# Newly placed tokens per expert: summed over the partitions by VectorE in place of a TensorE matmul

## What is computed

```
order = np.argsort(-flat)
for idx in order:
    tok, e = (int(idx) // E, int(idx) % E)
    if assigned[tok] >= 0 or counts[e] >= cap:
        continue
    assigned[tok] = e
    counts[e] += 1
```

## Time and profile before

| | us |
|---|---|
| median of 3 runs | 1106.54 |
| the profiled execution, its own time | 1105.22 |
| span of its instructions | 1103.1 |
| TensorE busy | 1041.5 |
| VectorE busy | 672.5 |
| one round, from a visit to the same visit of the next (497.10 to 610.20) | 113.1 |
| first route, TensorE mostly idle | about 145 to 190 |

### The profile page before, as it was taken

How to read it: one execution, slowest core, us unless ns; L and a number is a source line. 1 busy time by engine, 2 the same in 40 slices (tenths; PEclk the granted TensorE clock), 3 DMA queues, 4 the chain that set the end, 5 groups by cost and what they waited for, 6 DMA issues and landing times.

```text
span 1103.1 us, 20428 instructions
## 1 busy us (share of the span) xinstructions
PE 1041.5 (94%) x7340; PEld 971.1 (88%) x7340; DVE 672.5 (61%) x1965; ACT 344.3 (31%) x659; POOL 133.8 (12%) x159
## 2 busy tenths in 40 slices
PE   6999932999999999999999999999999999999996
PEld 5888821999999999999999999999999999999995
DVE  4665558877477647765677567755775477634211
ACT  3444422422243224322432234223412341224210
POOL 5554301033010011001100110011001100110001
PEclk9999965999999999999999999999999999999998
DMA  9999443312141113212321123122312230314000
GB/s 200 255 236 246 116 134 105 100 55 60 46 124 59 56 50 106 78 48 58 98 86 48 58 87 96 39 67 77 106 39 67 64 119 17 90 50 124 8 1 29
DMA packets 172988, 96.68 MB, mean 88 GB/s; under 512 B 80224, under 2 KB 158048, under 8 KB 172896
## 3 DMA queue, kind: packets, MB, share of 16 engines
q1 hardware_dynamic: 169056, 82.92, 28.7%
q0 software_dynamic: 3840, 12.59, 3.6%
HBM read 82.90 MB, written 12.58 MB: 87 GB/s over the span
## 4 chain that ended last, share of the span: by engine, by line
PE 82%; DVE 3%; issue 1%; POOL 0%; DMA 0%; DVEq 0%; POOLq 0%
PE bank L1200 21%; PE bank L1202 20%; PE bank L1201 20%; PE bank L1279 6%; PE bank L1280 6%; PE bank L1278 6%; PE bank L1195 1%; PE bank L1160 1%; DVE above L865 1%; PE bank L1187 0%; DVE onehot L1001 0%; DMA xg<-xrows,ids 0%; POOL out_dram L747 0%; PE bank L1166 0%; POOL xg L733 0%
## 5 line engine op out<-in xcount | busy, mean ns | idle before, releaser
L1200 PE MATMUL bank<-h2h,resident 128*128 128x384 f32 x768 | 261.2, 340 | 0.0
L1202 PE MATMUL bank<-h2h,resident 128*128 128x384 f32 x768 | 257.8, 336 | 0.0
L1201 PE MATMUL bank<-h2l,resident 128*128 128x384 f32 x768 | 257.4, 335 | 0.0
L1043 DVE TENSOR_TENSOR pf<-bank,gate 128x384 f32<-128x384 f32 x96 | 53.5, 557 | 159.9 <-PE bank L1202 158.9
L1200 PEld LDWEIGHTS bank<-h2h,resident 128*128 128x128 f32 x768 | 144.3, 188 | 3.0
L1201 PEld LDWEIGHTS bank<-h2l,resident 128*128 128x128 f32 x768 | 144.3, 188 | 2.9
L1202 PEld LDWEIGHTS bank<-h2h,resident 128*128 128x128 f32 x768 | 144.1, 188 | 0.0
L777 ACT ACTIVATE ring<-ring_raw 128x512 fp32r<-128x512 f32 x192 | 117.7, 624 | 65.8 <-DMA ring_raw<-in_moe_w_out_dram 41.0
L797 ACT ACTIVATE ph<-pf 128x384 fp32r<-128x384 f32 x96 | 50.4, 525 | 266.1 <-DVE pf L1043 266.1
L1052 DVE TENSOR_TENSOR ring<-ring_raw,ring 128x512 fp32r<-128x512 f32 x192 | 126.4, 684 | 0.0
L793 ACT ACTIVATE gate<-bank 128x384 f32<-128x384 f32 x96 | 47.1, 490 | 172.5 <-PE bank L1202 172.4
(11 more groups left out here) (175 smaller groups left out, 1689.9 us busy)
## 6 DMA issues: line engine op xcount, KB each, us to landing
ring_raw<-in_moe_w_dram SPq DMA_DIRECT2D x128, 256.0 KB, 2.9
ring_raw<-in_moe_w_out_dram SPq DMA_DIRECT2D x64, 256.0 KB, 2.9
qraw<-in_q_dram SPq DMA_DIRECT2D x24, 256.0 KB, 4.5
kraw<-in_k_dram SPq DMA_DIRECT2D x24, 256.0 KB, 5.1
vraw<-in_v_dram SPq DMA_DIRECT2D x24, 256.0 KB, 5.1
xrows<-xrow SPq DMA_DIRECT2D x24, 256.0 KB, 3.8
resident_raw<-in_moe_w_gate_dram SPq DMA_DIRECT2D x12, 256.0 KB, 4.5
resident_raw<-in_moe_w_val_dram SPq DMA_DIRECT2D x12, 256.0 KB, 4.6
```

What stands on the lines that cost most here:

```text
L1043: nc.vector.tensor_tensor(pf[:, f % 2, :], bank[2 * (f % 2) + 1][:, 0:CAP], gate[:, f % 2, :], ALU.mult).then_inc(p_ready, 1)
L1200: nc.tensor.matmul(ps, wh, xhi, start=start, stop=False)
L1201: nc.tensor.matmul(ps, wh, xlo, start=False, stop=False)
L1202: return nc.tensor.matmul(ps, wl, xhi, start=False, stop=stop)
```

## The change

The count step goes. Its DVE part and that of the rank step become one part, `V_RANK` = 8, with no matmul between them; the ids step is number 9, and there are 10 visits. The tokens placed by each partition (`fresh_sums`, 8 columns, padded with zeros to 32) are summed over the partitions by DVE: four turning sums (one for each quadrant of 32 partitions, each leaving one column of `quad_sums` over 32 partitions), a sum of the four columns (`total`), and four transposes of `total`, broadcast to 32x32, one into each quadrant (`spread`). The first 8 columns of `spread` then hold, on every partition, what the matmul with ones left in PSUM. The rank visit stands 7.4 us behind the tie visit in the column count, where it stood 10 us behind it; the one-hot parts and the ids visit move with it, 2.6 us earlier. By the same counting as above the lists become:

- TensorE: the tie visit as before; no count visit; the rank visit behind three quarters of value tile 4, before `out_products(3)`; the ids visit behind half of value tile 6.
- DVE: `product(2)`, `p_low(2)`, the new route part 8 (L959 to L969, the new instructions, L972 to L985), `product(3)`, `p_low(3)`, route part 9 (ids), `product(4)`, `p_low(4)`, three quarters of the one-hot tables, `product(5)`.

```diff
-        FIRST_CHAIN = 78
-        ROUTE_CHAIN = 120
+        FIRST_CHAIN = 88
+        ROUTE_CHAIN = 130
...
-        V_COUNT = V_TIE + 1
-        V_RANK = V_COUNT + 1
+        V_RANK = V_TIE + 1
...
-        visit_at += [visit_at[-1] + (n + 1) * LATE_GAP for n in range(2)]
+        visit_at += [visit_at[-1] + us(7.4)]
...
-        counted_fresh = sb("counted_fresh", [P, E], BF16)
+        fresh_sums = sb("fresh_sums", [P, RADIX], F32)
+        quad_sums = sb("quad_sums", [P, FOLD], F32)
+        total = sb("total", [P, 1], F32)
+        spread = sb("spread", [P, RADIX], F32)
...
+                    fill(fresh_sums[:, :], 0.0)
...
-                elif vis == V_COUNT:
+                elif vis == V_RANK:
...
-                    with nc.allow_low_precision(reason="counts up to 24"):
-                        nc.vector.reduce_sum(counted_fresh[:, :], fresh[:, :, :], AX_X).then_inc(route_ready, 1)
+                    link(nc.vector.reduce_sum(fresh_sums[:, 0:E], fresh[:, :, :], AX_X))
                     link(nc.vector.tensor_tensor(assigned[:, :, :], assigned[:, :, :], fresh[:, :, :], ALU.add))
                     link(nc.vector.reduce_sum(taken[:, :], over_experts(fresh[:, :, :]), AX_X))
                     link(nc.vector.tensor_tensor(unassigned[:, :], unassigned[:, :], taken[:, :], ALU.subtract))
-                elif vis == V_RANK:
-
-                    link(nc.vector.tensor_tensor(room[:, :], room[:, :], PS_K[:, 0:E], ALU.subtract))
+                    bins = slice(0, RADIX)
+                    for t in range(FOLD):
+                        last = nc.vector.tensor_reduce(quad_sums[bins, t:t + 1], fresh_sums[t * RADIX:(t + 1) * RADIX, :], axis=AX_X, op=ALU.add,
+                                                       apply_transpose=True)
+                        if t < FOLD - 1:
+                            count_only(last)
+                    link(last)
+                    link(nc.vector.reduce_sum(total[bins, :], quad_sums[bins, :], AX_X))
+                    for t in range(FOLD):
+                        last = nc.vector.transpose(spread[t * RADIX:(t + 1) * RADIX, :], total[bins, :].to_broadcast([RADIX, RADIX]))
+                        if t < FOLD - 1:
+                            count_only(last)
+                    link(last)
+                    link(nc.vector.tensor_tensor(room[:, :], room[:, :], spread[:, 0:E], ALU.subtract))
...
-                elif vis == V_COUNT:
-                    last = nc.tensor.matmul(PS_K[:, 0:E], ones[:, :], counted_fresh[:, :], start=True, stop=True)
```

More of the change, by code:

```diff
@@ L55, in retention_moe_glu_kernel @@
         PREP_CHAIN = 13
-        FIRST_CHAIN = 78
-        ROUTE_CHAIN = 120
+        FIRST_CHAIN = 88
+        ROUTE_CHAIN = 130
         CHAIN_START = PREP_CHAIN
-        TABLES = 7 + (TT - 1) + 6 + 3 + 3
+        TABLES = 7 + (TT - 1) + 7 + 3 + 3
         RING = 8
```

## The result

The changed kernel takes 1124.35 us (median of 4 runs, 1122.69 to 1124.91) against 1106.43 for the kernel before on the same chip: a ratio of 1.0161 (95% interval 1.0149 to 1.0173), 17.9 us slower. Forecast were 1121, in a range of 1117 to 1127. The profiled execution took 1122.69 us, its span 1120.7; before they were 1105.22 and 1103.1.

A forecast was written before the change was run, and what follows sets the result against it. TensorE's own work was taken to bound the kernel. First route 2.18, steady rounds 9.0 and round 0 3.4 made +14.6 us on a median of 1106.54: 1121 us, with 8 in 10 between 1117 and 1127.

The forecast's parts named there:

- E: Work added on DVE by the new sums and transposes in each route: 2.18 us, bounds 1.75 to 2.72.
- the turning sum's 0.94: Time taken for the four new DVE transposes, from four turning sums of the same block size: 0.94 us.
- The first route: Before round 0: the removed matmul was hidden and gives nothing back, so all of E is added, +2.18 us.
- The steady rounds: Rounds 1 to 6: TensorE stalls 1.65 us before `out_products(3)`, less 0.15 for a visit; 1.50 each, +9.0 in all.
- The slack of 2.94: Steady round before the change: `p_low(3)` ended 2.94 us before `out_products(3)` started.
- Term C: Round 0: `out_products(3)` start 3.55 us later, less 0.15 for the visit; +3.4 us, bounds 3.0 to 4.6.
- a bound for the transposes only: Round 0: if POOL holds the transposes as well, the round's added time is 4.6 us.
- TensorE's clock falls at each stall: Rival: each of the seven stalls in the rounds loses 1.5 us more at half clock, time 1132 us; chance 6%.
- Hidden work: Rival: DVE's work ahead of `product(3)` grows by less than the slack, TensorE does not stall, 1106 us; chance 4%.
- The chance of 95% for slower: Whole kernel: 95% that it measures slower than before by more than 2.2 us.

The follow-up runs named there:

- f3: The changed kernel with the count of the first route alone made by the matmul with ones again; 1123.39 us, ratio 1.0156.
- f1: The changed kernel with sums and rank part moved behind `p_low(3)`, first half still ahead of `product(3)`, rank visit 10 us behind the tie visit; 1109.3 us.
- f4: The changed kernel with four more transposes of the same kind into a spare tile in every route; 1131.66 us, ratio 1.0226.
- f2: The changed kernel with the rank visit 10 us behind the tie visit again, behind `out_products(3)`; 1124.38 us, ratio 1.0158.
- second execution: The changed kernel run once more as it is, against the kernel before; 1124.21 us, ratio 1.0158.
- g1: f1 with the count of the first route alone made by the matmul with ones, as in f3; 1107.87 us, ratio 1.0013.

## Why the prediction was right, and what in it was off

*What bounds it; E.* Right, and each term to 0.01 where it was worked from rows of the same form: E was 2.18 and is 2.15. For the plain transposes I had chosen the turning sum's 0.94 between 0.51 and 1.48; they took 0.93. The estimate by the Trainium skill ("VectorE: DVE Perf Modes", "The TRN2 errata"), E 1.84, was low: small transposes of 32x32 do not start closer than 0.23 us to each other, and an instruction took 0.20.

*The first route.* Right: +2.16. The count's matmul had been hidden, so its removal gave nothing back; f3 shows the stretch go back to 29.11.

*The steady rounds.* The mechanism was right in each step. The slack of 2.94 ahead of `out_products(3)` was used up by 4.4 us of new work ahead of `product(3)`; f1 takes the work from there and the stall is gone, f4 adds 0.90 and the round grows by 0.93, f2 shows that `p_low(3)` and not the rank visit sets the end. 1.50 was forecast and 1.59 measured. Of the 0.09 more, 0.05 went to the restart: the first output matmul behind the pause takes 0.30 to the next in place of 0.23, and the nine take 2.14 in place of 2.09. The other few hundredths are not placed.

*Round 0, the step that was mis-sized.* "Term C = +3.4" was 5.54. Its pause was right (3.24 later, 3.55 forecast; POOL held neither L986, which DVE reached at 257.76 as POOL's instruction ended at 257.70, nor the transposes). What it left out is the clock: 2.3 us lost at half rate behind the pause; and in the second execution the second pause was 1.9 in place of 0.70, mostly POOL's hold of `p_low(3)`, a hold that I had as a bound for the transposes only. I had the rival "TensorE's clock falls at each stall", gave it 6% and let it hold for all seven or for none, on the ground that a pause of 1.43 us at 11.70 had done no harm. That ground was empty. The windows show a clock of 1.00 for that stretch, but the four transposes behind the pause took 1.11 us and four of the same form at 15.48 took 0.66: TensorE ran at half pace there before the pause and behind it (those at 8.33 took 1.09), so the pause could do no harm. The trace of before has no pause of more than 0.7 us within a stretch at full clock, and could say nothing for or against the rival. The runs show it in between: never in twelve steady rounds of the changed kernel (pauses of 0.26 and 1.11) or in six of f2 (1.7), in two of six of f4 (1.2 and 1.1); in round 0 of f1 and not of g1, behind the same pause of 1.77; and in round 0 of the changed kernel (twice), f2, f3 and f4, with 2.6 to 4.8 us of pauses. What decides it at pauses of 1 to 2 us stays open. The Trainium skill ("TensorE: Matmul & The Clock Gate", "Why this matters for your kernels") warns of long pauses only; by that rule no single pause here but the 3.6 of f2's round 0 should have mattered, and round 0 of f1 speaks against it, with 3 us at half clock behind a pause of 1.77.

*The range.* 1124.35 lies in it, but the room above 1121 had been made for dearer transposes and for POOL. The transposes cost what was forecast. It was the clock that used the room, and that it fits is luck.

*The rivals.* Hidden work needed E below 0.59: E was 2.15. The chance of 95% for slower stood on two rows, the slack and the turning sums, and both held.

## What to carry to other kernels

A matmul and the wait for it can be free when the waiting engine has other work to do meanwhile; before it is replaced, look whether the step behind it began with a wait at all (here it began 0.03 us behind DVE's own work). What an engine's added work costs is not its time but its time less the slack of the next result that the bound engine wants from it, so a part that merges two steps also pulls the second one ahead of whatever stood between them; moving the same instructions behind that result took back 15 of 18 us. A pause on TensorE may be paid twice, once as waiting and once at half clock. Whether a pause left the clock alone is read from the pace of the same matmuls before and behind it, not from the clock column alone: here that column showed 1.00 for a stretch at half pace.

## What the runs showed of the hardware

- A VectorE transpose of 32x32 fp32 takes 0.20 us, four in a row 0.90, like four turning sums of the same block; two of either never overlapped, where two small elementwise instructions with no wait between them started 0.09 apart.
- The transposes took 0.90 also while POOL ran its subtraction beside them (256.59 to 257.49 against 256.40 to 257.70), but an elementwise instruction of DVE that ran beside a POOL instruction begun ahead of it was stretched, L966 from 0.36 to 0.98 and in f1 `p_low(3)` from 0.56 to 1.48. The Trainium skill ("GPSIMD Engine Reference", "1. Specifications") says that GpSimd shares its SBUF interface with VectorE and names two-input instructions as contended; both rows agree.
- The granted clock fell to 0.50 behind single pauses of 1.77 (f1) and 3.6 us (f2) and behind pairs of 1.9 and 0.7 (after) and of 1.2 and 1.1 (two rounds of f4), and stayed there for 3 to 7 us. It stayed at 1.00 behind pauses of 1.77 (g1), of 1.7 (f2, six times) and of 1.2 and 1.1 (f4, four rounds).
- After the idle stretch of the first route the clock came back 2.8 us behind TensorE's restart at the earliest (before, after) and 5.7 at the latest (f4).
